# Table loads, the last exponentials, the rounding of weight rows and one mixed sum are placed elsewhere in a fused attention, mixer and gated-convolution kernel

## The reference

```python
# 1. banded attention: 8 heads of 64, window of 96 tokens and 8 global ones
scores = q @ k.T / 8 + bias                  # masked outside the band
a = exp(scores - max); a = a / (sum(a) + 1e-9)
x = a @ v                                    # [2, 768, 512]
# 2. a mixer over tokens and channels
theta = x @ w_theta
y = w_tok_r @ (x * cos(theta)) + w_tok_i @ (x * sin(theta))
u = x + y
x = u + maximum(u @ w_ch, 0)
# 3. a gated convolution over tokens (3 taps), 1024 hidden channels
h = maximum(x @ w_in, 0)
gate = 1 / (1 + exp(-conv3(h, conv_w)))
out = (h * gate) @ w_out
```

## Time and profile before

| | |
|---|---|
| median of 3 runs | 394.95 us (394.83 to 395.25) |
| profiled execution, its time | 394.86 us |
| profiled execution, its span | 393.1 us |
| TensorE matmul busy | 385.1 us, 98% of the span |
| VectorE, ScalarE, GpSimd busy | 251.8, 223.7, 139.9 us |
| granted TensorE clock | 1.00 |

### The profile page before, as it was taken

How to read it: one execution, slowest core, us unless ns; L and a number is a source line. 1 busy time by engine, 2 the same in 40 slices (tenths; PEclk the granted TensorE clock), 3 DMA queues, 4 the chain that set the end, 5 groups by cost and what they waited for, 6 DMA issues and landing times.

```text
span 393.1 us, 6248 instructions
## 1 busy us (share of the span) xinstructions
PE 385.1 (98%) x2214; PEld 337.7 (86%) x2214; DVE 251.8 (64%) x633; ACT 223.7 (57%) x441; POOL 139.9 (36%) x119
## 2 busy tenths in 40 slices
PE   7999999999999999999999999999999999999996
PEld 3888889888788888888898899998999899899985
DVE  5977777765787899998998744665553343443410
ACT  3777777774776785424544352855863644644531
POOL 2079999992345200400000072033852232232230
PEclk9999999999999999999999999999999999999999
DMA  7998879244000362412312430003300200200022
GB/s 230 419 410 351 291 286 368 115 198 88 0 0 3 107 242 80 161 48 74 82 40 69 159 107 0 3 1 117 98 3 0 80 2 1 80 2 0 2 80 80
DMA packets 15728, 43.98 MB, mean 112 GB/s; under 512 B 4560, under 2 KB 4816, under 8 KB 15696
## 3 DMA queue, kind: packets, MB, share of 16 engines
q1 hardware_dynamic: 15696, 43.57, 31.3%
HBM read 32.16 MB, written 11.40 MB: 111 GB/s over the span
## 4 chain that ended last, share of the span: by engine, by line
PE 91%; ACT 4%; DVE 2%; issue 1%; DMA 1%; ACTq 0%
PE bank L514 29%; PE bank L666 19%; PE bank L723 17%; PE bank L561 9%; PE bank L546 6%; PE bank L533 5%; PE bank L646 3%; PE bank L626 1%; PE bank L572 1%; PE bank L679 1%; ACT h_sb L998 1%; DMA woutraw<-w_out_in 1%; ACT pr L796 1%; DVE bank L1454 0%; ACT bank L1006 0%
## 5 line engine op out<-in xcount | busy, mean ns | idle before, releaser
L666 PE MATMUL bank<-b_ops,a_ops 128*128 128x512 f32 x324 | 75.5, 391 | 0.0
L514 PE MATMUL bank<-vT,win 128*128 128x386 f32 x384 | 73.3, 340 | 0.9 <-ACT h_sb L998 0.9
L514 PEld LDWEIGHTS bank<-vT,win 128*128 128x128 f32 x384 | 68.3, 188 | 3.4 <-issue 1.0
L666 PEld LDWEIGHTS bank<-b_ops,a_ops 128*128 128x128 f32 x324 | 60.5, 188 | 12.3
L723 PE MATMUL bank<-wout,g 128*128 128x512 f32 x288 | 69.5, 390 | 0.0
L488 POOL TENSOR_TENSOR g<-gf,g 128x384 fp32r<-128x384 f32 x32 | 32.6, 1019 | 94.2 <-ACT g L1018 94.2
L723 PEld LDWEIGHTS bank<-wout,g 128*128 128x128 f32 x288 | 53.9, 188 | 9.7
L1454 DVE SCALAR_TENSOR_TENSOR bank<-h_sb,convw,bank 128x384 f32<-128x384 f32 x32 | 19.9, 622 | 65.9 <-ACT bank L1006 65.9
L998 ACT ACTIVATE h_sb<-bank 128x386 f32<-128x386 f32 x32 | 15.8, 494 | 51.8 <-PE bank L514 48.6
L796 ACT ACTIVATE pr<-biased,small 128x232 f32<-128x232 f32 (+1 forms) x96 | 39.6, 464 | 1.3 <-DVE small L1126 1.3
L807 ACT ACTIVATE pT<-bank 128x512 f32<-128x512 f32 (+1 forms) x48 | 26.9, 561 | 19.8 <-PE bank L561 18.1
(11 more groups left out here) (98 smaller groups left out, 572.8 us busy)
## 6 DMA issues: line engine op xcount, KB each, us to landing
qk_sb<-qk_laid SPq DMA_DIRECT2D x7, 792.0 KB, 9.4
v_sb<-v_laid SPq DMA_DIRECT2D x6, 780.0 KB, 8.7
w_raw<-w_tok_laid SPq DMA_DIRECT2D x6, 768.0 KB, 13.7
a_kept<-stage SPq DMA_DIRECT2D x6, 768.0 KB, 4.0
a_ops<-a_kept SPq DMA_DIRECT2D x6, 768.0 KB, 4.9
a_kept<-stage SPq DMA_DIRECT2D x9, 384.0 KB, 2.8
a_ops<-a_kept SPq DMA_DIRECT2D x9, 384.0 KB, 3.1
out<-ob SPq DMA_DIRECT2D x12, 256.0 KB, 2.1
```

The source lines that it names most:

```text
L514: last = pe.matmul(dst, w[a], m[b], start=(i == 0 and j == 0), stop=(i == n - 1 and j == 2))
L666: last = pe.matmul(y_bank(s)[:], a_ops[:, slot, hi, blk, :], b_ops[:, side, blk, lo, :], start=(blk == 0 and j == 0), stop=(blk == NT - 1 ...
```

## The change

On ScalarE, a sine of one element per partition is taken right after `high_x(1)`, and a sigmoid of one element right after `high_v(11)`; both write to a new tile `warm` that nothing reads. The compiler's table loads go with them. At the end of attention `exps(46)` stands ahead of `copy_p(44)` and `exps(47)` ahead of `copy_p(45)`. All eight `high_w_out(f)` stand behind `first_steps(5 + f)` instead of `first_steps(4 + f)`. On VectorE, `add_mix(12)` stands ahead of `gate(2)`.

```diff
+        warm = at("warm", [P, 1], F32, 0.90625)
...
-                for u in range(NU):
+                for u in range(NU - 4):
                     copy_p(u)
-                    if u + 2 < NU:
-                        exps(u + 2)
+                    exps(u + 2)
+                for u in (NU - 4, NU - 3):
+                    exps(u + 2)
+                    copy_p(u)
+                copy_p(NU - 2)
+                copy_p(NU - 1)
                 high_x(0)
...
             high_x(1)
+            act.activation(warm[:], half_pi[:], ACT.Sin)
             for t in range(TT):
...
             high_v(11)
+            act.activation(warm[:], half_pi[:], ACT.Sigmoid)
...
             high_v(15)
+            first_steps(5)
             high_w_out(0)
-            for f in range(1, 6):
-                first_steps(4 + f)
+            for f in range(1, FB):
+                first_steps(5 + f)
                 high_w_out(f)
-            for n in range(6 + CB, NH):
+            for n in range(FB + 5, NH):
...
                 gates(n)
-                if n < 12:
-                    high_w_out(n - 4)
...
             hidden(2)
-            hidden(3)
+            conv(3)
             add_mix(12)
+            gate(2)
             add_mix(13)
```

## The result

The changed kernel takes 391.25 us (median of 5 runs, 391.13 to 391.95), the kernel before 395.15 us in the runs beside it (394.83 to 395.47); the ratio is 0.9907, 95% interval 0.9896 to 0.9918. So it is faster by 0.9%, where 391.1 us had been forecast: 3.9 us between these medians, 3.7 by the ratio. The profiled execution took 391.25 us, its span is 389.5 us, 3.6 us shorter than that of before.

A forecast was written before the change was run, and what follows sets the result against it. TensorE, nearly always busy, bounds the kernel; removing its six waits gives 0.35 + 0.85 + 2.6 = 3.8 us, from 394.86 to 391.1. Likeliest range 390.8 to 391.5 (0.68); 8 in 10: 390.7 to 392.3.

The forecast's parts named there:

- Waits read on the weight loads: Six TensorE waits near the change, measured as idle time of weight loads, not matmul rows; 3.8 us in all.
- the matmul rows' idle time: Rival: the gates give only 1.36 us instead of 2.6, so 2.55 in all, 392.3 us; chance 0.05.
- Exponentials, 0.35: End of attention: the transpose of unit 46 no longer waits for its exponentials; gain 0.35 us, bounds 0 and 0.4.
- Sine table, 0.85: Angle tiles: with the load moved ahead of turns(0), theta(4)'s wait goes; gain 0.85 us, bounds 0.6 and 0.85.
- Sigmoid table, sum and w_out, 2.6: First gate tiles: four waits go, 0.56 + 0.53 + 0.55 + 0.98 us; bounds of the stage 1.5 and 2.65.
- The sum ahead of the gate, nothing: VectorE, add_mix(12) ahead of gate(2): the old order makes low_v(12) perhaps 0.1 us later; by itself priced at nothing.
- The one-element function, 0.3 taken: ScalarE ahead of turns(0): price of the one-element sine, bounded by 0.64 us above, taken as 0.3.
- GpSimd's queue, nothing, 0.5 us to spare: Tile loop: each low_g about 2 us later behind low_w_out; gates have 0.5 us to spare, so priced at nothing.
- short chain: Rival: places with 0.3 us to spare fail or angles meet the store; 391.5 to 392.5 us; chance 2 in 10.
- The two places of 0.3 us to spare: Gate tiles: the third channel product and hidden(8), each expected to be ready 0.3 us before TensorE arrives.
- The slower rival: w_out's DMA landing late holds relu(6) and GpSimd's rounding; a loss only past 8 us, at 9 us 395.8; chance 0.03.
- the waits would be taken over by others: Rival: other TensorE waits of the same length replace those removed, so the change does nothing, 394.9 us; chance 0.04.

The follow-up runs named there:

- The two single tests: Changed kernel without the one-element sine: 392.61 us, ratio 0.9933; kernel before with the one-element sine alone: 394.44 us, ratio 0.9982.

## Why the prediction was right

*Waits read on the weight loads.* Right. The sum over them was 3.8 us, the span lost 3.6 and the median 3.9; the matmul rows' idle time would have given 2.55. The Trainium skill's warning on matmul busy time (Perfetto Trace Analysis, Identifying the Most-Contended Engine) is borne out by this.

*Exponentials, 0.35.* theta(0) starts 0.40 us earlier, at 90.05 for 90.45, though the first scores start 0.04 us later (6.68 for 6.64). From those on it is 0.43 to 0.44 us. The mechanism was right, the term a little too small and just past its upper bound of 0.4; where the 0.08 beyond the wait come from was not looked into.

*Sine table, 0.85.* theta(4) starts 1.27 us earlier, of which 0.40 were there at theta(0): 0.87. The two single tests give 0.80 and 0.75. Right.

*Sigmoid table, sum and w_out, 2.6.* The mechanism was right and the size 0.2 us too large: between hidden(0) and output(0, 0) 3.65 - 1.25 = 2.40 us went. By its parts, it is 0.57 for 0.56 up to the first product, 0.48 for 0.53 from there to the third, and 1.35 for 1.53 from there to output(0, 0), past the two hidden tiles. What was missing in the term: the weight loads of a product that comes behind a wait are sent in 4.12 us, those of one that doesn't in 4.18 or 4.19, and 2.06 to 2.08 against 2.12 for twelve. Each such product gives back some 0.05 us of the wait ahead of it. This term was 0.2 too large and that of the exponentials 0.1 too small, which offset each other in part: the sum owes some of its closeness to that.

*The sum ahead of the gate, nothing.* Right, and its undoing shows it.

*The one-element function, 0.3 taken.* It is 0.20.

*GpSimd's queue, nothing, 0.5 us to spare.* Right: measured against output(0, 0) the low halves from that of tile 4 to that of tile 10 came 1.0 to 1.8 us later (2 had been taken), no gate waited for them, and one tile further the queue closes the loop.

*The rivals.* No short chain remained. The two places of 0.3 us to spare have 0.5 us ahead of the third product and, by an estimate from the row of 48 weight loads, 0.3 ahead of hidden(8). The slower rival, a late DMA of w_out, did not come up: its first row was rounded at 267.16 without waiting. That the waits would be taken over by others is refuted by the weight loads, which wait for nothing.

Left open is whether the clock is what changes the pace of the fillers. The recorded clock does not show it, and no run separates it from another cause.

## What to carry to other kernels

Where one engine is nearly always busy, list its few waits on the weight loads, follow each to what is queued ahead of the late instruction, and move that into a wait which the same engine has anyway; a table load is moved by a one-element call of its function. Check the new place for its cover and for the queues of the other engines: here one tile later gave 1.3 to 1.4 us, and a second tile on top lost 9.7. What an edit gives depends on which others are in, so price a chain as a whole and undo one edit at a time.

## What had not been expected of the hardware

A load of the table cost its 1.28 us here and no drain beside it: load and one-element call repeat every 1.50 us. The start of the program differs by up to 1.0 us between executions of kernels that are the same up to theta(0) (its weight loads start between 89.90 and 90.92 us), mainly by the pace of the first matmuls, 0.22 or 0.43 us for 512 columns. Nine fillers with two more behind them and no gap between gave the narrowest runs, 390.64 to 390.94 us, in four runs only.
